# Delta-rule attention and two feed-forward layers on one core: another table of steps, with the next group's key products spread behind the 32-wide ones

## The reference

```python
batch, n_heads, seq, head_dim = (4, 8, 768, 48)
k_n = k / (np.linalg.norm(k, axis=-1, keepdims=True) + 1e-06)
for t in range(S):
    y[:, :, t] = np.einsum('bhd,bhde->bhe', q[:, :, t], state)
    v_old = np.einsum('bhde,bhd->bhe', state, kt)
    state = state + bt[:, :, :, None] * np.einsum('bhd,bhe->bhde', kt, vt - v_old)
...
h = np.maximum(x @ w_in, 0.0)              # 3072x384 @ 384x2048
x = h * h @ w_out                          # 2048x384
gate = 1.0 / (1.0 + np.exp(-(x @ w_gate))) # 384x1536
y = gate * (x @ w_val) @ w_out2            # 1536x384
```

## Time and profile before

| | us |
|---|---|
| median of three runs | 1157.03 |
| the profiled execution | 1154.64 |
| its span | 1152.9 |
| stage 0 (to the first block) | 102.7 |
| stage 1 | 128.4 |
| stages 2 to 5 | 109.6, 109.3, 109.3, 101.3 |
| stage 6 and the second layer | 492.3 |
| PE busy | 1041.9 (90%) |
| DVE busy, ACT busy | 587.7, 439.0 |

### The profile page before, as it was taken

The page is one execution under the profiler, slowest core; times in us unless marked ns, Lnnn a source line. Parts: engine busy times, 40 slices in busy tenths (PEclk is TensorE's granted clock), DMA queues, the critical chain, the costliest instruction groups (busy, mean ns, idle before and its releaser), DMA issues.

```text
span 1152.9 us, 22982 instructions
## 1 busy us (share of the span) xinstructions
PE 1041.9 (90%) x9885; PEld 559.0 (48%) x9885; DVE 587.7 (51%) x1100; ACT 439.0 (38%) x752; POOL 12.6 (1%) x27
## 2 busy tenths in 40 slices
PE   2487589889988998899889999999999999999997
PEld 1285256446644664466446544444444444444443
DVE  7857944792489159716952445424233342422422
ACT  4544145425434443445244498222222222132221
POOL 0000000000000000000000000000000000000000
PEclk7559689988989998899889999999999999999999
DMA  9414002300230042004200050101001010010000
GB/s 299 74 43 71 0 2 46 67 28 2 71 42 29 2 94 45 1 16 70 110 2 2 1 193 27 55 1 55 0 0 55 0 55 0 0 55 0 27 0 27
DMA packets 54850, 48.10 MB, mean 42 GB/s; under 512 B 45424, under 2 KB 49392, under 8 KB 54384
## 3 DMA queue, kind: packets, MB, share of 16 engines
q1 hardware_dynamic: 54336, 46.67, 15.9%
q10 hardware_dynamic: 432, 0.23, 0.1%
HBM read 37.45 MB, written 9.44 MB: 41 GB/s over the span
## 4 chain that ended last, share of the span: by engine, by line
PE 74%; DVE 21%; issue 2%; ACT 1%; DMA 1%; SPq 0%; DVEq 0%; POOL 0%; POOLq 0%
PE psum L525 59%; DVE attn L875 4%; DVE attn L873 4%; DVE attn L893 3%; PE psum L401 3%; PE psum L463 2%; PE psum L476 2%; PE psum L436 2%; PE psum L451 2%; PE psum L413 2%; DVE work L915 2%; DVE work L934 1%; PE psum L425 1%; DVE attn L880 1%; DVE attn L834 1%
## 5 line engine op out<-in xcount | busy, mean ns | idle before, releaser
L525 PE MATMUL psum<-work,w 128*128 128x512 f16 x1728 | 411.0, 395 | 34.6 <-DVE work L915 30.5
L525 PE MATMUL psum<-work,attn 128*128 128x512 f16 x1944 | 419.9, 379 | 0.1
L525 PEld LDWEIGHTS psum<-work,attn 128*128 128x128 f16 x1944 | 190.1, 98 | 229.8 <-DVE work L934 0.6
L525 PEld LDWEIGHTS psum<-work,w 128*128 128x128 f16 x1728 | 167.3, 101 | 245.5 <-DVE work L915 39.0
L606 ACT ACTIVATE work<-work 128x512 f16<-128x512 f32 (+1 forms) x264 | 156.2, 624 | 147.2 <-DVE work L1096 139.9
L1096 DVE SCALAR_TENSOR_TENSOR work<-psum,work 128x512 f32<-128x512 f32 x72 | 49.8, 692 | 269.7 <-PE psum L525 258.8
L606 ACT ACTIVATE attn<-psum 32x512 f32<-32x512 f32 (+4 forms) x168 | 81.5, 500 | 107.5 <-PE psum L401 54.8
L606 ACT ACTIVATE work<-psum 128x512 f32<-128x512 f32 x96 | 57.0, 594 | 152.1 <-PE psum L525 151.8
L915 DVE SCALAR_TENSOR_TENSOR work<-work 128x512 f16<-128x512 f16 x96 | 66.2, 690 | 85.2 <-ACT work L606 83.8
L606 ACT ACTIVATE work<-psum,scal 128x512 f32<-128x512 f32 x72 | 49.4, 687 | 138.5 <-PE psum L525 137.8
L909 DVE TENSOR_TENSOR attn<-attn,psum 64x384 f32<-64x384 f32 x48 | 26.5, 552 | 86.4 <-PE psum L476 68.0
(11 more groups left out here) (77 smaller groups left out, 584.9 us busy)
## 6 DMA issues: line engine op xcount, KB each, us to landing
attn<-in_kt SPq DMA_DIRECT2D x24, 192.0 KB, 4.1
attn<-in_v SPq DMA_DIRECT2D x6, 768.0 KB, 4.8
attn<-in_kn SPq DMA_DIRECT2D x6, 768.0 KB, 7.4
x_spill<-work SPq DMA_DIRECT2D x6, 768.0 KB, 3.6
xt<-x_spill SPq DMA_DIRECT2D x6, 768.0 KB, 4.9
y_out<-work SPq DMA_DIRECT2D x6, 768.0 KB, 3.6
attn<-in_qt SPq DMA_DIRECT2D x20, 192.0 KB, 4.7
work<-in_w_out SPq DMA_DIRECT2D x1, 3072.0 KB, 21.6
```

The lines of the kernel that those rows point to most:

```text
L525: m = mm(dst, x, z, start=first and i == 0, stop=last and i == len(a) - 1)
```

## The change

All positions move into one table, `PLACE`, with `OTHER` for stages 0 and 1. From stage 2 on qk stands at 2, 4, 7 and 9, to_rows at 2, mid at 6, off at 6 and 7, kk of the next group at 7, 9, 9 and 14, ks at 7 and 16, dr 12 and 16, yy and su 13 and 19, xt 13 and 25, lanes and norms 15, start 16, maximum 27. `column_steps` now reckons for each step what room DVE has beside its other work, from the step after start to the step before to_rows. The gram of keys is cut: each 64x64 product becomes two with 32 columns of weights, the second with the two halves of its moving columns exchanged, so that both diagonal 32x32 blocks lie in the same columns of `gp` and one transpose of all 128 partitions puts them on lanes. `middle` reads the block that has changed place. SP also waits for the last qk fill of a stage before it loads keys into the buffer.

```diff
-L_NORM, L_DIAG, L_COEF, L_START, L_COL = 0, 3, 4, 12, 14
+L_NORM, L_DIAG, L_COEF, L_START, L_COL = 0, 1, 2, 10, 12
...
+PLACE = dict(rows=2, scale_v=7, mid=(6, 6), off=(6, 7), qk=(2, 4, 7, 9), ks=(7, 16), dr=(12, 16), grow=(13, 19), xt=(13, 25), xmax=27, xscale=30, xsplit=31, kk=(7, 9, 9, 14), lanes=15, norm=15, start=16)
+OTHER = {
+    0: dict(mid=(8, 8), off=(8, 13), qk=(11, 11, 16, 22), ks=(10, 19), dr=(13, 20), grow=(16, 22), xt=(16, 25), xmax=27, xscale=31, xsplit=31, kk=(24, 26, 26, 27), lanes=28, norm=29, start=32, first_in=(10, 15, 18), first_out=(19, 21, 26, 26), small=(12, 15, 17, 21)),
+    1: dict(rows=9, scale_v=19, mid=(12, 12), off=(14, 14), qk=(-2, 1, 2, 4), ks=(19, 21), dr=(19, 24), grow=(20, 25), xt=(20, 29), xmax=29, xscale=31, xsplit=31, kk=(14, 15, 19, 19), lanes=20, norm=20, start=20),
+}
...
+EVACUATION = {"qk": 1.4, "ks": 0.6, "su": 1.1}
+STEP_US = 1.5
+FIRST_US = 1.75
+def other_work(s, step):
+    us = sum(EVACUATION.get(kind, 0.0) for kind, *_ in FILL_AT.get((s, step), []))
+    for name, cost in (("rows", 4.3), ("scale_v", 3.2), ("xmax", 1.8), ("xscale", 1.0), ("xsplit", 4.0), ("lanes", 2.2),
+                       ("start", 4.0)):
+        if s < GROUPS and step == place(s, name):
+            us += cost
+    if step % 2 == 0 and 2 <= step <= 2 * N1:
+        us += 0.7
+    if step == 0 and s > 1:
+        us += 2.4
+    return us
...
-    room = [((g - 1, step), 1.0) for step in range(COLS_FROM + late(g - 1), STEPS)] if g > 1 else []
-    room += [((g, step), 1.5) for step in range(0, COLS_TO + late(g))]
-    cost = [2 * (BL - 1 - j) * (j + 1) + 240 for j in range(BL - 1)]
+    start, end = place(g - 1, "start") + 1, place(g, "rows")
+    steps = [(g - 1, step) for step in range(start, STEPS)]
+    steps += [(g, step) for step in range(0, end)]
+    spare = 0.0
+    room = []
+    for at in steps:
+        spare += STEP_US - other_work(*at) if at[0] else FIRST_US
+        room.append(max(0.0, spare))
+        spare = min(spare, 0.0)
+    cost = [2 * (BL - 1 - j) * (j + 1) + 300 for j in range(BL - 1)]
...
                     wait_full(sp, "ks", s, 1, 1)
+                    wait_full(sp, "qk", s, 1, 1)
...
-                for j, i in itertools.product(range(HALF), range(2)):
+                for j, h, i in itertools.product(range(HALF), range(1 if kind == "qk" else 2), range(2)):
...
-                    last = mm(to[steps_of(i), CH * j:CH * (j + 1)], k, pq[rows, u, i, :] if kind == "qk" else k,
-                              start=True, stop=True)
+                    if kind == "qk":
+                        last = mm(to[steps_of(i), columns], k, pq[rows, u, i, :], start=True, stop=True)
+                    else:
+                        moving = k.rearrange("p (h t) -> p h t", t=BL)[:, ::-1, :] if h else k
+                        last = mm(to[part_of(i, h), columns], k[:, part_of(0, h)], moving, start=True, stop=True)
...
-                    last = mm(to[CH * i:CH * i + BL, BL * j:BL * (j + 1)], gp[rows, u, 0:BL], e_s[rows, u, BL:CH],
+                    last = mm(to[CH * i:CH * i + BL, BL * j:BL * (j + 1)], gp[rows, u, BL:CH], e_s[rows, u, BL:CH],
...
-            def to_lanes(g, n):
+            def to_lanes(g):
...
-                rows, b = ((slice(0, P), 0), (slice(BL, 2 * BL), BL), (slice(3 * BL, P), BL))[n]
-                lane(V.transpose(lane_g[rows].rearrange("p (s t) -> p t s", t=BL),
-                                 gp[rows, :, b:b + BL].rearrange("p u t -> p t u")), g, L_NORM + n)
+                lane(V.transpose(lane_g.rearrange("p (s t) -> p t s", t=BL),
+                                 gp[:, :, 0:BL].rearrange("p u t -> p t u")), g, L_NORM)
```

More of the change, by code:

```diff
@@ L128, in column_steps @@
             at += 1
[L129 to L130 removed]
+            edge += room[at] * scale
+        out.setdefault(steps[at], []).append(j)
         used += x
@@ L731, in stage @@
                         hidden_square_lo(k, s - 1)
-                    if 0 < s < GROUPS and step == ROWS_AT + 1 + late(s):
+                    if 0 < s < GROUPS and step == place(s, "rows") + 1:
                         place_e(s)
```

117 lines of the change are left out of this document (47 added, 70 removed).

## The result

The changed kernel takes **1097.53 us**, the median of four runs (1088.92 to 1100.69), beside 1156.86 us of the kernel before on the same chip: a ratio of 0.948, 95% interval 0.944 to 0.952. The profiled execution is the longest of the four, 1100.69 us, with a span of 1098.9. The forecast was 1112 us with a range of 1090 to 1132; between the two profiled executions the change gained 54 us of span (1152.9 to 1098.9) where 45 were expected, and by the medians 59.

The account below looks back on a forecast made before the run. PE was taken as the bound, its waits and the slow matmuls behind them as winnable: 11.2 (stages 0 and 1) + 44.5 (stages 2 to 5) - 11.3 (grams) = 44.4, say 45 us, giving a median of 1112 us, range 1090 to 1132.

Parts of the forecast that it names:

- Stages 2 to 5 without the grams: Stages 2 to 5: PE's waits and the slow matmuls behind them go, 46.5 us less 0.5 a stage, 44.5 us.
- The 1.46 and the 3.57: PE waits in us, some 20 us after a stage's last-block wait and before mid's products; both were to go.
- The slack of 2 us ahead of mid: From the end of hidden block 15 to mid: DVE needs 16.9 us, PE 19 us, leaving 2 us.
- The half microsecond taken for small waits: Stages 2 to 5: 0.5 us a stage given back for small waits in steps with four to six fills.
- The grams, +0.94 us a fill and +15 us in all: Cut gram fills for groups 2 to 5: 16 more matmuls make a fill 2.0 us; 16 fills on the path.
- The rival with four tiles abreast and +0: Gram fills: four tiles run abreast, so the cut adds +0 instead of +0.94 us a fill; 1091 us, 15%.
- Stages 0 and 1: To the end of stage 1: 5.8 + 6.1 + 3.0 - 3.75 = 11.2 us gained, start of stage 1 unchanged.
- One lane transpose: One transpose instead of three takes 4.3 us off DVE in a stage, beside PE there: nothing gained.
- the clock drops of the dense steps: Rival: small matmuls at steps 7, 9 and 13 drop the clock or delay evacuations, 2 to 4 us a stage; 1120 to 1132, 20%.
- the +18 case: Rival: columns catch up with DVE or x's scale is late; two waits return in four stages, +18, 1130 us, 5%.
- The slower case: Rival: each gram matmul waits for the whole one before, fill 7.0 us, 1223 us; decides from 3.9 a fill; 3%.
- the main case: The prediction's own case for the whole kernel, 1104 to 1120 us, given 55%.

Follow-up runs that it names:

- the experiment: Changed kernel with only the gram fill's loop nesting altered, qk included: two places of the array in turn 1108.42 us, one place 1171.49 us.

## Why the prediction was right, and where it was not

**Stages 2 to 5 without the grams**: right. Predicted were 10.2, 12.5, 12.5 and 9.3 us less, 44.5 together; measured 10.8, 13.6, 11.4 and 9.7, together 45.5. Stage 5's 0.97 us, taken from the trace of before as the price for every boundary, is what stages 2 to 4 now show. The 1.46 and the 3.57 went, and the cold matmuls with them. That the columns hold this up is shown by putting them late: 33.7 us come back. The slack of 2 us ahead of mid was right too: in stage 3 to_rows ends at 333.42 us and mid starts at 335.62. (The prediction's words count five blocks there, which with its other terms make 17.2 us; the trace has six, and they make its 19.) The half microsecond taken for small waits was right as well: 0.36 us, once a stage. Stage 4 lacks 2.2 us for a cause that the steps did not have, a pause and the low clock behind it (timeline of PE in the changed kernel):

```profile
433.89 0.92 PE L450 MATMUL psum<-attn 32*32 32x32 f32 x47 [0.36 <-ACT attn L631]
435.22 0.47 PE L450 MATMUL psum<-attn 32*32 32x32 f32 x17 [0.41 <-issue]
435.62 3.37 PE L550 MATMUL psum<-work,w 128*128 128x512 f16 x9
```

**The grams, +0.94 us a fill and +15 us in all**: the step that failed. It was taken "because the two windows differ in nothing but the moving columns", and from them came that the next matmul waits until the second pass of the one before starts. So each matmul more was priced at 0.059 us, the price of the 64-wide ones; the cut fill shows 1.03 us for 32, which is 0.032 each. What the runs put in its place: the pace is not one rule between neighbours, it depends on which places of the array follow one another. In a whole fill two places take turns, so 34 ns a record there is a figure for two in turn. Both narrow windows stand at the start of a fill, and why only one matmul had started in one of them no run shows. The cut fill goes round four places and costs 1.03 us. The rival with four tiles abreast and +0, given 15%, was right: it said 1091. The Trainium skill's rule that different tiles work in parallel (TensorEngine Tiling (Array Packing), Key Properties) agrees with the trace here, by 1.03 against 1.73 us for the same 64 records with two places in turn. By the medians 11 us are lost with two, and 74 with one in the fills of both kinds. With two the clock in stage 0 had the short shape; against the changed kernel's run of 1088.9 us the loss is 19.5, near the 16.8 of 24 fills at 0.70 us. What sets the 16 ns a record with four in turn stays open (see the experiment).

**Stages 0 and 1**: predicted 11.2 us less, of which 3.75 were the dearer grams of group 2, so 15 without them; measured 8.4. The opening's grams were put 3.0 us later for the cut and came 4 later for another cause, mainly the pause of 3.37 us. The start of stage 1, taken as unchanged at 102.7, came at 106.8: the profiled execution has the low clock up to 90 us and the pause of 4.18 us after it. With the gap before mid filled, it comes at 96.0. Mid of stage 1, set at 145.3, came at 149.05, late by the same 4 us. The wait at the end of stage 1, left at about 4 us, is 4.17.

**One lane transpose, "beside PE: nothing"**: right for the old table (1152.0 us with cut and transposes alone, 3.6 less), and wrong as a reading of the new one, where it is what keeps 18.7 us. The sum is not off by it, since it was made with one transpose; but its 34 against 39 to 40 us left 5 us of slack for DVE ahead of the split, and the runs show some 2.

**The other rivals.** Of the clock drops of the dense steps the profile shows one, in stage 4 (2.2 us), behind the pauses above; stage 2's clock of 0.97 is its start, where 27 matmuls behind the 4.17 us wait take 8.65 us instead of 6.00, as the prediction had it. That is far less than the 1120 to 1132 of that rival. Columns or split late again, the +18 case, is what the late columns show (+33.7) and the three transposes behind the ks copies (+13). The slower case needed every gram matmul to wait for the whole of the one before, 7.0 us a fill. Matmuls in one place do follow more slowly, but at 3.11 us a fill. The kernel with them took 1171 us, some 16 more than the kernel before beside it, though below the 3.9 us a fill from which the prediction let this case decide (its 22 fills and 66 us make 4.1); its qk fills had grown by 0.75 us too, and two kk fills met the low clock at 4.81 us each, so where the point lies for kk alone isn't shown.

Taken together, 45.5 from stages 2 to 5 and 8.4 from stages 0 and 1 are the 54 us of the profiles. The sum was out by 9 of 45: it took 15 us off the gain for the grams that they didn't cost, it had 1 us too little for the rest of stages 2 to 5, and 6.6 too much for stages 0 and 1. These errors offset each other in part, which is luck. The median of 1097.53 us lies in the stated range, but outside the 1104 to 1120 of the main case, and nearer to the first rival's 1091. Of the 14.5 us between forecast and median the sum has 9; the other 5.6 are that the profiled execution stood 2.4 us below the median before the change and 3.2 above it after, with the long shape of stage 0's clock.

## What to carry to other kernels

Issue small matmuls so that consecutive ones lie in different places of the array, and read how they follow each other from a window in which the same place comes again; the order of one loop, which serves both kinds of gram, was worth 74 us here. An engine that is a third idle can still have little slack on each stretch between two things that are awaited from it: two more transposes of 2.1 us and the whole grams cost 3.6 us in one table, nothing of it in the middle stages, and 18.7 us in the next. A wait can be worth itself plus slow matmuls behind it (4.13 and 2.3 us at the ends of the stages before); look at the clock behind each wait of TensorE, and compare spans only when it rose at the same places in both.

## What the runs showed that was not expected

- Matmuls with 32 columns of weights and 64 moving fp32 columns: 16 ns a record with four places in turn, 27 with two, 49 with one, at full clock. Whole grams, 64 columns of weights: 34 ns with two in turn, 57 with one.
- PE can stand still with nothing awaited that the profile shows: at the opening for 2.6 to 3.8 us while loads kept the DMA engines full, and for 1.4 when they were put off.
- In stages 2 to 5 a pause of PE of 0.41 us next to another of 0.36 was followed by nine matmuls in 3.37 us instead of 2.03 and by a granted clock of 0.83 from 437 to 445 us, while 0.36 alone, in stage 3, and 0.36 next to 0.26, in stage 2, were followed by none. With grams in one place the clock fell to 0.50 for 12 us, 19 us behind the last pause.
- The same work shows two shapes of TensorE's clock in stage 0: group 1's first gram fill starts at 82 to 85 us in one and at 88 to 92 in the other. That can explain most of the changed kernel's spread of 1089 to 1101 us. Twelve more idle matmuls, which add 2.4 us of PE work, take 9 us off the median and most of the spread.
